# One stage of a fused attention and two-MLP kernel: the attention rounds start their second half one step earlier, and five weight loads move up in a DMA queue

## The chip, the cores and the metric

The kernel runs on one core of one Trainium2 chip. Its time is device microseconds (us) of one execution; the number quoted for a version is the median of its runs. Times "at 158.97" count from the first instruction of the profiled execution.

## What is computed

Three steps follow one another on 4608 tokens of 512 features. `setup_inputs` scales the random inputs; the reference is, cut to what matters:

```python
# attention, separately in every chunk of 64 positions; q, k, v are (8, 8, 576, 64)
scores = matmul(q_c, k_c.T) / sqrt(64)
attn = exp(scores - max(scores)); attn = attn / (sum(attn) + 1e-9)
x = matmul(attn, v_c)                    # -> (4608, 512)
# first MLP, 512 -> 1536 -> 512
x = (sigmoid(x @ w_gate) * (x @ w_val)) @ w_out
# second MLP, 512 -> 2048 -> 512
h = x @ w_in
g = where(h >= 1, h, where(h <= -1, 0, (h + 1) ** 2 / 4))
out = g @ w_out2
```

## The kernel before

All five engines run programs of their own, written out by hand, and meet only at semaphores. Every matmul product is made of three matmuls, since each operand is split into a rounded high part and the low rest.

**First stage** (before 207 us). The first two groups of 384 tokens (t = 0, 1) go through the first MLP with weights that lie in on-chip memory. Per group there are 12 units, and a unit has three **thirds**: a gate product, a val product and an output product, of 12 matmuls each. The steps are numbered `third = (t * C1 + n) * 3 + j`, 0 to 71, and TensorE, ScalarE and VectorE all walk the same numbers. Between the products lie 12 **rounds** of attention (rounds 4 to 15), one for every five thirds. For a round, TensorE makes the scores (`scores`, L649) at the head of a third with `third % 5 == 4`; VectorE subtracts the maximum in that third (`shift`, L1337 and L1340) and divides by the sum in the next (`normalize`, L1348 to L1354); ScalarE takes the exponential (L967). TensorE transposes the probabilities (`transpose_probs`, L660) at `third % 5 == 2`, ScalarE copies them back (`copy_probs_t`, L977), and TensorE multiplies them by v (`mix`, L682) at `third % 5 == 3`. ScalarE then copies the result (`make_x_hi`, L989, in rounds 4 to 7, `save_x`, L1004, in the others) and triggers the next load of v; for rounds 4 to 7 VectorE makes the low part (`make_x_lo`, L1365). In the third with j == 1 VectorE also makes the gated product of the val product of that third (`gated`, L1380 and L1383); its instructions stand in the order shift, normalize, make_x_lo, gated.

**Passes.** From then on 11 passes (MLP1 = 5 of the first MLP, MLP2 = 6 of the second) work on 768 tokens each, with a scheme that makes one product of 2 by 2 blocks out of seven smaller ones. Its operands are sums and differences of blocks: of x (`x_sum`, then `combo_hi` on ScalarE and `combo_lo` on VectorE, L1055 and L1422) and of the weights. A pass has 12 (later 8) units of seven products and then an output stage of 21 (later 28) split pairs (`split_hi` L1145, `split_lo` L1535, TensorE L828 to L830). Passes 0 to 3 carry eight rounds of attention each for the pass behind them. Before the first product of kind 6 of pass 0, TensorE waits for a copy of ScalarE (`copy_chain`, L1068), which stands behind all seven `combo_hi` of that pass in ScalarE's order, and the last of these needs the fourth `x_sum`.

**Weights of the passes.** GpSimd makes the combined and split weights from raw pieces, piece by piece (`prepare`): four operands per piece for the first 18 pieces, 72 in all, each a subtraction (L598), a rounded copy (L605) and the rest (L607). They go into three buffers in turn (from operand 12 on `prep_early`), and from there to device memory. From device memory they come back by loads into a ring of five slots (`load_ring`, L486); two loads make a unit. Ring slots 0 to 4 lie over weights of the first stage, so load n (n < 5) waits for val product 6 + n of t = 1.

All of this is issued by **one queue, SP**, in one written order. `store_prepared` (L452) waits for GpSimd's operand, stores it, and issues loads of the next raw piece before and after (L437). Whatever stands behind a waiting instruction waits too. In pass 0 one load_ring is followed by two, one or two stores, by turns, until all 72 are out (`many`). Load 24 is the first of the output stage of pass 0. The buffers `prep_early` lie where split pairs 2 and 3 are written, so the third `split_hi` of pass 0 waits until every one of the 72 stores has landed.

Of the kernel before, what the change touches and what calls it, by code (L numbers as in the profile page):

```python
# [21 lines left out]
NR = 4  # L22
# [111 lines left out]
def attention_and_mlps(nc, q_k, v, w_gate, w_val, w_out, pieces, out):  # L134
# [4 lines left out]
    with ExitStack() as ctx:  # L139
# [94 lines left out]
        def bank(b):  # L234
            return banks[:, b, 0:N]
# [191 lines left out]
        def _(sp):  # L427
# [88 lines left out]
            for b in (0, 1, 3, 2):  # L516
                load_raw(0, b)
            prepared = 0
            for upto, n in ((35, 0), (38, 1), (41, 2), (44, 3), (46, 4)):
                while prepared < upto:  # L520
                    if prepared % 4 == 0:
                        for _ in range(2 if prepared < 16 else 1):
                            if stored < PIECES_1:
                                store_kept(stored)
                                stored += 1
                    store_prepared(prepared)
                    prepared += 1
                load_ring(0, n)
# [91 lines left out]
        def _(pe):  # L620
# [32 lines left out]
            def transpose_probs(a):  # L653
                way = FIRST[a] if a < NR else FIRST[-1]
                pe.wait_ge(probs_ready, a + 1)
                if 2 <= a < NR:
                    pe.wait_ge(probs_t_copied, a - 1)
                tr = way.tr if a < NR else bank(0)
                for b in range(GROUP // 2):
                    last = pe.transpose(tr[:, b * P:(b + 1) * P], way.probs[:, b * P:(b + 1) * P], ident[:, :])  # L660
                last.then_inc(probs_t_done, 1)
# [243 lines left out]
            for t in range(TILES):  # L905
                for n in range(C1):
                    for j in range(3):
                        third = (t * C1 + n) * 3 + j
                        if third % 5 == 4 and third // 5 < 12:
                            scores(NR + third // 5)  # L910
                        if third % 5 == 2 and 0 < third // 5 <= 12:
                            transpose_probs(NR + third // 5 - 1)
                        if third % 5 == 3 and 0 < third // 5 <= 12:
                            mix(NR + third // 5 - 1)
                        t_next, n_next = t + (n + 1) // C1, (n + 1) % C1
                        if j == 2:
                            add_out(t, n)
                        elif t_next < TILES:
                            (gate, val)[j](t_next, n_next)
                        else:  # L920
                            unit(0, 0, order(0)[j])
# [25 lines left out]
        def _(act):  # L947
# [27 lines left out]
            def copy_probs_t(a, way=FIRST[-1]):  # L975
                act.wait_ge(probs_t_done, a + 1)
                act.activation(way.probs, way.tr if a < NR else bank(0), ACT.Copy).then_inc(probs_t_copied, 1)  # L977
# [217 lines left out]
            for t in range(TILES):  # L1195
                for n in range(C1):
                    for j in range(3):
                        third = (t * C1 + n) * 3 + j
                        if third % 5 == 4 and third // 5 < 12:
                            exponentiate(NR + third // 5)  # L1200
                        if third % 5 == 2 and 0 < third // 5 <= 12:
                            copy_probs_t(NR + third // 5 - 1)
                        if third % 5 == 3 and 0 < third // 5 <= 12:
                            a = NR + third // 5 - 1
                            if a < 2 * NR:
                                make_x_hi(a)
                            else:
                                save_x(a)
                        m = t * C1 + n + 1
                        if j == 0 and m < TILES * C1:  # L1210
                            make_gate(m)
                        if j == 1 and m < TILES * C1:
                            make_g_hi(m)
                        if j == 1 and t == TILES - 1:
                            if n == 6:
                                combo_part(0, 0)
                            if n == 9:
                                combo_part(0, 1)
                            if n == 10:
                                combo_part(0, 2)  # L1220
                                combo_part(0, 3)
                                combo_part(0, 4)
                            if n == 11:
                                combo_part(0, 5)
                                combo_part(0, 6)
                if t == TILES - 1:
                    copy_chain(0, 0, 1)
                save_x2(t)
                store_x2(t)
# [75 lines left out]
        def _(dve):  # L1305
# [269 lines left out]
            for t in range(TILES):  # L1575
                for n in range(C1):
                    for j in range(3):
                        third = (t * C1 + n) * 3 + j
                        if third % 5 == 4 and third // 5 < 12:
                            shift(NR + third // 5)  # L1580
                        if third % 5 == 0 and 0 < third // 5 <= 12:
                            normalize(NR + third // 5 - 1)
                        if third % 5 == 3 and 0 < third // 5 <= NR:
                            make_x_lo(NR + third // 5 - 1)
                        m = t * C1 + n + 1
                        if j == 1 and m < TILES * C1:
# [180 lines left out]
```

## Time and profile before

| what | value |
|---|---|
| median of 3 runs | 1682.48 us (1680.63 to 1684.82) |
| profiled execution: its own time / its span | 1680.63 us / 1678.8 us |
| TensorE busy | 1630.9 us, 97% |
| VectorE, ScalarE, GpSimd busy | 66%, 48%, 26% |
| granted TensorE clock, mean | 0.997 |
| TensorE idle before ring products (L806), 0 to 460 us, for DMA | 5.3 us in 3 waits |

A row of the trace in order of time gives the start, the duration, the engine, the line and the operation, and in brackets how long the engine was idle before it and what released it. Matmuls overlap: each is 0.33 us long, but they start 0.17 us apart at full clock. GpSimd is called POOL, VectorE DVE, ScalarE ACT, TensorE PE, and SPq is the SP queue.

### The profile page before, as it was taken

How to read it: one execution, taken by the hardware profiler on the slowest of the kernel's cores; microseconds unless marked ns; L12 is line 12 of the kernel's file. 1: busy time of each engine (PE TensorE's matmuls, PEld its weight loads, DVE VectorE, ACT ScalarE, POOL GpSimd, SP SyncE). 2: the span in 40 equal slices, each digit the busy share in tenths (PEclk: the TensorE clock that was granted, in tenths of full speed). 3: DMA queues.
4: the chain of work that ended last, by engine and by line, in shares of the span. 5: the costliest groups of instructions: out<-in, count | busy, mean ns of one | idle time of the engine just before them, and what ended most of it. 6: DMA issues, size and time to landing. Idle time of an engine off the chain costs nothing.

```text
span 1678.8 us, 29062 instructions
## 1 busy us (share of the span) xinstructions
PE 1630.9 (97%) x11028; PEld 1586.9 (95%) x11028; DVE 1105.7 (66%) x1607; ACT 805.1 (48%) x1301; POOL 439.3 (26%) x582
## 2 busy tenths in 40 slices
PE   6999999999999999999999999999999999999999
PEld 6999988999989999999999999999999999999999
DVE  5444556576586659456744858669579578688585
ACT  2222333354444445344433556466475475575563
POOL 7877766203460454145134000000000000000000
PEclk9999999999999999999999999999999999999999
DMA  7799899889998998998899887787777787778675
GB/s 193 243 297 322 265 331 337 286 291 326 340 325 298 330 344 309 318 322 320 293 350 330 294 302 286 243 303 284 249 300 278 238 311 267 266 300 277 236 290 171
DMA packets 153386, 489.50 MB, mean 292 GB/s; under 512 B 18080, under 2 KB 68768, under 8 KB 124192
## 3 DMA queue, kind: packets, MB, share of 16 engines
q1 hardware_dynamic: 134368, 457.76, 78.3%
q10 hardware_dynamic: 18880, 29.89, 5.7%
q8 instruction: 88, 1.44, 0.3%
q14 instruction: 50, 0.41, 0.1%
HBM read 406.32 MB, written 81.26 MB: 290 GB/s over the span
## 4 chain that ended last, share of the span: by engine, by line
PE 66%; DMA 11%; POOL 8%; issue 5%; DVE 3%; SPq 1%; ACT 1%; POOLq 0%; DVEq 0%; ACTq 0%
PE banks L806 12%; PE banks L808 11%; PE banks L807 11%; PE banks L828 10%; PE banks L830 10%; PE banks L829 10%; POOL raw L598 3%; POOL prep_early L607 2%; DMA ring<-w_in_split 2%; DMA out_dram<-y 2%; DMA w_in_split<-prep_b 2%; DMA w_in_split<-prep_a 2%; POOL prep_early L605 2%; DMA raw<-pieces_dram 1%; DVE split_lo L1535 1%
## 5 line engine op out<-in xcount | busy, mean ns | idle before, releaser
L806 PE MATMUL banks<-combo_hi,ring 128*128 128x384 f32 x1512 | 519.1, 343 | 18.0 <-DMA ring<-w_in_split 8.6
L808 PE MATMUL banks<-combo_hi,ring 128*128 128x384 f32 x1512 | 507.8, 336 | 0.0
L807 PE MATMUL banks<-combo_lo,ring 128*128 128x384 f32 x1512 | 507.3, 336 | 0.0
L828 PE MATMUL banks<-split_hi,ring 128*128 128x384 f32 x1092 | 366.2, 335 | 6.8 <-DVE split_lo L1535 4.9
L830 PE MATMUL banks<-split_hi,ring 128*128 128x384 f32 x1092 | 364.9, 334 | 0.0
L829 PE MATMUL banks<-split_lo,ring 128*128 128x384 f32 x1092 | 364.9, 334 | 0.0
L806 PEld LDWEIGHTS banks<-combo_hi,ring 128*128 128x128 f32 x1512 | 285.2, 189 | 28.0 <-DMA ring<-w_in_split 11.9
L807 PEld LDWEIGHTS banks<-combo_lo,ring 128*128 128x128 f32 x1512 | 285.4, 189 | 0.0
L808 PEld LDWEIGHTS banks<-combo_hi,ring 128*128 128x128 f32 x1512 | 285.2, 189 | 0.0
L1068 ACT ACTIVATE chain<-banks 128x384 f32<-128x384 f32 x324 | 156.6, 488 | 226.9 <-PE banks L808 221.5
L1535 DVE TENSOR_TENSOR split_lo<-g,split_hi 128x768 fp32r<-128x768 f32 x234 | 231.4, 993 | 35.7 <-ACT split_hi L1145 33.9
L1145 ACT ACTIVATE split_hi<-g 128x768 fp32r<-128x768 f32 x234 | 193.2, 842 | 128.6 <-PE banks L830 69.8
L828 PEld LDWEIGHTS banks<-split_hi,ring 128*128 128x128 f32 x1092 | 205.0, 188 | 10.9 <-issue 9.6
L829 PEld LDWEIGHTS banks<-split_lo,ring 128*128 128x128 f32 x1092 | 205.0, 188 | 0.0
L830 PEld LDWEIGHTS banks<-split_hi,ring 128*128 128x128 f32 x1092 | 205.0, 188 | 0.0
L598 POOL TENSOR_TENSOR raw<-raw 128x256 f32<-128x256 f32 x136 | 116.6, 857 | 54.9 <-DMA raw<-pieces_dram 41.7
L605 POOL CAST prep_a<-raw 128x256 fp32r<-128x256 f32 x56 | 30.9, 552 | 295.0 <-DMA w_in_split<-prep_a 159.4
L1422 DVE TENSOR_TENSOR combo_lo<-x_raw,combo_hi 128x768 fp32r<-128x768 f32 x77 | 78.3, 1019 | 17.0 <-ACT combo_hi L1055 17.0
L1118 ACT ACTIVATE r<-h,half 128x384 f32<-128x384 f32 x48 | 29.6, 617 | 86.6 <-DVE h L1457 86.6
L690 PE MATMUL banks<-x_tile,weights 128*128 128x384 f32 x192 | 67.5, 352 | 0.3 <-DVE x_tile L1359 0.2
L1055 ACT ACTIVATE combo_hi<-x_raw 128x768 fp32r<-128x768 f32 x77 | 63.9, 833 | 3.0 <-issue 3.0
L967 ACT ACTIVATE probs<-probs 128x384 f32<-128x384 f32 x45 | 23.6, 525 | 86.8 <-DVE probs L1340 86.8
(121 smaller groups left out, 2110.1 us busy)
## 6 DMA issues: line engine op xcount, KB each, us to landing
ring<-w_out_split SPq DMA_DIRECT2D x119, 1024.0 KB, 6.6
ring<-w_in_split SPq DMA_DIRECT2D x108, 1024.0 KB, 6.8
ring<-w_in_split SPq DMA_DIRECT2D x108, 768.0 KB, 7.1
ring<-w_out_split SPq DMA_DIRECT2D x35, 512.0 KB, 5.6
raw<-pieces_dram SPq DMA_DIRECT2D x136, 128.0 KB, 5.1
tile_in<-q_k_dram ACTq DMA_DIRECT2D x44, 384.0 KB, 6.2
w_in_split<-weights SPq DMA_DIRECT2D x36, 256.0 KB, 3.7
w_in_split<-prep_early SPq DMA_DIRECT2D x36, 256.0 KB, 3.5
```

The lines of the kernel that those rows point to most:

```text
L598: pool.tensor_tensor(into, *less, op=ALU.subtract).then_inc(prep_summed, 1)
L690: pe.matmul(ps, w_lo, x_hi(par, j), start=(j == 0), stop=False)
L806: pe.matmul(ps, w_lo, hi, start=first and k == 0, stop=False, skip_group_check=more)
L807: pe.matmul(ps, w_hi, lo, start=False, stop=False, skip_group_check=more)
L808: last = pe.matmul(ps, w_hi, hi, start=False, stop=k == 1, skip_group_check=more)
L828: pe.matmul(ps[:, j, :], w_lo, hi, start=first and k == 0, stop=False, skip_group_check=more)
L829: pe.matmul(ps[:, j, :], w_hi, lo, start=False, stop=False, skip_group_check=more)
L830: last = pe.matmul(ps[:, j, :], w_hi, hi, start=False, stop=end, skip_group_check=more)
L1068: act.activation(buf[:, u % 2, :], x_bank(p, u), ACT.Copy).then_inc(copied, 1)
L1145: act.activation(split_hi[:, at % 4], g_part(p, i, kp), ACT.Copy).then_inc(split_hi_ready, 1)
L1422: dve.tensor_tensor(combo_lo[:, i - 1], x_part(i), combo_hi[:, i - 1].bitcast(F32), op=ALU.subtract).then_inc(combo_lo_ready, 1)
L1535: dve.tensor_tensor(split_lo[:, b], g_part(p, i, kp), split_hi[:, b].bitcast(F32), op=ALU.subtract)\
```

## The change

Two edits. On the SP queue, the first five ring loads stand behind 28, 31, 34, 36 and 38 stores of prepared operands instead of 35, 38, 41, 44 and 46; the stores that no longer stand ahead of them follow in pass 0 with the same pattern, which then ends at ring load 25 instead of 20. In the first stage, transposes, mix, the copies behind each and `make_x_lo` move one third earlier; scores, shift, exponential and normalize stay.

```diff
--- before.py
+++ after.py
@@ -516,7 +516,7 @@
             for b in (0, 1, 3, 2):
                 load_raw(0, b)
             prepared = 0
-            for upto, n in ((35, 0), (38, 1), (41, 2), (44, 3), (46, 4)):
+            for upto, n in ((28, 0), (31, 1), (34, 2), (36, 3), (38, 4)):
                 while prepared < upto:
                     if prepared % 4 == 0:
                         for _ in range(2 if prepared < 16 else 1):
@@ -908,9 +908,9 @@
                         third = (t * C1 + n) * 3 + j
                         if third % 5 == 4 and third // 5 < 12:
                             scores(NR + third // 5)
+                        if third % 5 == 1 and 0 < third // 5 <= 12:
+                            transpose_probs(NR + third // 5 - 1)
                         if third % 5 == 2 and 0 < third // 5 <= 12:
-                            transpose_probs(NR + third // 5 - 1)
-                        if third % 5 == 3 and 0 < third // 5 <= 12:
                             mix(NR + third // 5 - 1)
                         t_next, n_next = t + (n + 1) // C1, (n + 1) % C1
                         if j == 2:
@@ -1198,9 +1198,9 @@
                         third = (t * C1 + n) * 3 + j
                         if third % 5 == 4 and third // 5 < 12:
                             exponentiate(NR + third // 5)
+                        if third % 5 == 1 and 0 < third // 5 <= 12:
+                            copy_probs_t(NR + third // 5 - 1)
                         if third % 5 == 2 and 0 < third // 5 <= 12:
-                            copy_probs_t(NR + third // 5 - 1)
-                        if third % 5 == 3 and 0 < third // 5 <= 12:
                             a = NR + third // 5 - 1
                             if a < 2 * NR:
                                 make_x_hi(a)
@@ -1580,7 +1580,7 @@
                             shift(NR + third // 5)
                         if third % 5 == 0 and 0 < third // 5 <= 12:
                             normalize(NR + third // 5 - 1)
-                        if third % 5 == 3 and 0 < third // 5 <= NR:
+                        if third % 5 == 2 and 0 < third // 5 <= NR:
                             make_x_lo(NR + third // 5 - 1)
                         m = t * C1 + n + 1
                         if j == 1 and m < TILES * C1:
```

## Rows read from the trace of the kernel before

**Rows 1.** The page: busy time of each engine, share of the span, instructions.

```profile
PE 1630.9 (97%) x11028; PEld 1586.9 (95%) x11028; DVE 1105.7 (66%) x1607; ACT 805.1 (48%) x1301; POOL 439.3 (26%) x582
```

**Rows 2.** TensorE in time order: start us, us, engine, line, operation.

```profile
39.62 0.33 PE L729 MATMUL banks<-g_hi,weights 128*128 128x384 f32 x1
...
41.70 0.33 PE L690 MATMUL banks<-x_tile,weights 128*128 128x384 f32 x1
```

**Rows 3.** TensorE in time order, at the end of the first stage.

```profile
213.81 0.66 PE L806 MATMUL banks<-combo_hi,ring 128*128 128x384 f32 x1 [2.66 <-DVE combo_lo L1422]
...
220.22 0.40 PE L806 MATMUL banks<-combo_hi,ring 128*128 128x384 f32 x1
```

**Rows 4.** Waits of TensorE, 280 to 320 us: us in total, times, longest.

```profile
PE banks L806 <- DMA ring<-w_in_split: 5.3, 3, 2.0
```

**Rows 5.** TensorE in time order, late in pass 0.

```profile
289.65 0.45 PE L806 MATMUL banks<-combo_hi,ring 128*128 128x384 f32 x1 [1.96 <-DMA ring<-w_in_split]
...
302.55 0.52 PE L808 MATMUL banks<-combo_hi,ring 128*128 128x384 f32 x1
```

**Rows 6.** The SP queue in time order: a store and ring loads.

```profile
163.23 0.33 SPq L452 DMA_DIRECT2D w_in_split<-prep_early  x1
...
181.65 0.33 SPq L486 DMA_DIRECT2D ring<-w_in_split  x1
...
217.21 1.79 SPq L486 DMA_DIRECT2D ring<-w_in_split  x2
```

**Rows 7.** TensorE in time order: scores and transposes of the rounds, waits in brackets.

```profile
43.87 0.58 PE L649 MATMUL banks<-tile_in 64*64 64x64 f32 x24
...
51.57 0.55 PE L660 MATMUL banks<-ident,probs 128*128 128x128 f32 x3 [0.67 <-DVE probs L1354]
...
96.05 0.58 PE L649 MATMUL banks<-tile_in 64*64 64x64 f32 x24 [0.49 <-DVE x_tile L1365]
...
146.44 0.58 PE L649 MATMUL banks<-tile_in 64*64 64x64 f32 x24
...
158.97 0.58 PE L649 MATMUL banks<-tile_in 64*64 64x64 f32 x24
...
165.83 0.49 PE L660 MATMUL banks<-ident,probs 128*128 128x128 f32 x3
```

**Rows 8.** VectorE in time order: probabilities ready, and two gated products.

```profile
99.44 0.75 DVE L1354 TENSOR_TENSOR probs<-probs,row_sum 128x384 f32<-128x384 f32 x1
...
151.36 1.00 DVE L1354 TENSOR_TENSOR probs<-probs,row_sum 128x384 f32<-128x384 f32 x1
...
164.62 0.56 DVE L1354 TENSOR_TENSOR probs<-probs,row_sum 128x384 f32<-128x384 f32 x1
168.52 0.56 DVE L1380 SCALAR_TENSOR_TENSOR g_full<-act_buf,banks 128x384 f32<-128x384 f32 x1 [3.33 <-PE banks L692]
...
198.76 0.55 DVE L1380 SCALAR_TENSOR_TENSOR g_full<-act_buf,banks 128x384 f32<-128x384 f32 x1 [5.83 <-PE banks L692]
```

**Rows 9.** VectorE in time order: the same operation in two stretches.

```profile
207.32 3.98 DVE L1422 TENSOR_TENSOR combo_lo<-x_raw,combo_hi 128x768 fp32r<-128x768 f32 x3
...
339.73 0.95 DVE L1422 TENSOR_TENSOR combo_lo<-x_raw,combo_hi 128x768 fp32r<-128x768 f32 x1
```

**Rows 10.** ScalarE in time order, before TensorE goes on.

```profile
213.20 0.47 ACT L1068 ACTIVATE chain<-banks 128x384 f32<-128x384 f32 x1
```

**Rows 11.** GpSimd in time order: first and last of 24 finished operands.

```profile
229.06 0.73 POOL L607 TENSOR_TENSOR prep_early<-raw,prep_early 128x256 fp32r<-128x256 f32 x1
...
304.32 0.73 POOL L607 TENSOR_TENSOR prep_early<-raw,prep_early 128x256 fp32r<-128x256 f32 x1
```

**Rows 12.** One tile (raw), its DMAs from 220 to 310 us.

```profile
DMA to landing us min/median/max: 3.3/6.3/8.8
```

**Rows 13.** ScalarE in time order, start of the output stage of pass 0.

```profile
330.25 2.32 ACT L1145 ACTIVATE split_hi<-g 128x768 fp32r<-128x768 f32 x3 [2.57 <-DVE g L1469]
```

**Rows 14.** DMA issues, 220 to 310 us: size of one, median us to landing.

```profile
w_out_split<-prep_early SPq DMA_DIRECT2D x24, 256.0 KB, 5.0
```

## Prediction

> **What bounds the kernel now.** I read the page first. TensorE is busy for 97% of the span [rows 1], so only a stop of TensorE, or a spell of its lower clock, can be won or lost. The stages (forty-slice table, windows) put nearly all of its idle time that this change can touch before 330 us. There I read TensorE in order of time, with the idle time ahead of each instruction, and beside it the queues that feed it. Four facts matter.
>
> First, in the first stage TensorE runs without a gap from third to third; a third is twelve matmuls, 41.70 - 39.62 = 2.08 us [rows 2]. Second, where pass 0 begins it stops for 2.66 us and then runs at half rate until 220.22 [rows 3]. Third, late in pass 0 it waits three times for ring loads, 5.3 us in all [rows 4], the first at unit 8 [rows 5]. These loads are late because the SP queue issues them behind stores of prepared operands, and those wait for GpSimd. Fourth, the first ring load goes out at 181.65 [rows 6] although its data is wanted only when pass 0 begins, so loading it earlier is worth nothing by itself. What the edit of the queue really does is change how many stores stand ahead of each later load.
>
> The profiled execution took 1680.63 us (span 1678.8 and 1.8 around it), the lowest of the three; the median is 1682.48. I make the sum against the profiled execution and add it to the median. Differences under 0.3%, some 5 us, are about what a measurement of this kernel cannot tell from none.
>
> **Part 1: transposes, mix and their copies one third earlier.** Per round these are three transposes and 24 small matmuls on TensorE, one copy of the transposed probabilities, two copies of the mix and the trigger of the next v load on ScalarE, and for four rounds two subtractions on VectorE. Nothing is added or removed, so the only price is waiting. The transposes need the probabilities, and VectorE's place for making them does not move.
>
> Today the transposes start 165.83 - 158.97 = 6.86 us after the scores start [rows 7]; one third less leaves 4.78 us. The twelve rounds fall into three kinds, by the place of the scores in the unit of three thirds.
> - Scores ahead of a val product (rounds 4, 7, 10 and 13). VectorE must do the gated product of that val before it normalizes. Probabilities are ready at 164.62 + 0.56 = 165.18, the transposes would be wanted at 158.97 + 4.78 = 163.75: a stop of 1.4 [rows 7, 8]. Three rounds are like this (my readings of the others: 1.4 and 1.5), 4.3 in all. Round 4 is worse: wanted at 43.87 + 4.78 = 48.65, and its transposes start at 51.57, as soon as the probabilities are there [rows 7], so 2.9 instead of the 0.67 paid today, 2.2 more.
> - Scores ahead of the output product (four rounds): wanted at 146.44 + 4.78 = 151.22, ready at 152.36, 1.1 us; the four give 1.1, 1.0, 1.1 and 0.6, so 3.7 in all.
> - Scores ahead of a gate (four rounds): wanted at 96.05 + 4.78 = 100.83, ready at 100.19 [rows 7, 8]. Free, with 0.6 to spare.
>
> TensorE's queue is served in order, so behind the waiting transposes stand the gate, val and output products, and they all move. The mix still comes a third after the transposes, so the 0.5 us copy between them stays hidden: free. If that cover went, each round would pay up to the copy. The earlier mix removes two waits of the scores for x (0.49 of them in [rows 7]) and a small one, 1.0 together. Part 1: +2.2 + 4.3 + 3.7 - 1.0 = **+9.2 us**.
>
> A stop may also cost clock. After the 2.66 stop TensorE ran 18 matmuls in 220.22 - 213.81 = 6.4 us, half of its rate, where 3.1 is the price at the upper level (2.4 GHz): about 3 lost [rows 2, 3]. Round 4's stop would be 2.9 long. But stops of 1.96 and less did not all do this: after 289.65 the rate stayed, and only near 302.55 are there starts 0.32 us apart, about ten of them, 1.5 lost [rows 5]. Bounds for round 4 are 0 and 3; I take **+1.5**, since the nearest row dropped but in a stretch with another wait right behind it. For the 1.0 to 1.5 us stops I take nothing.
>
> **Part 2: the start of pass 0.** After the change SP has issued 28 stores at 163.23 [rows 6] and then waits, in ring load 0, for a val product that ends at about 168.5 [rows 8], now some 8.7 later, at 177. Behind that wait stand the stores, the loads of raw pieces and the kept operands; GpSimd waits for stores (three buffers) and for raw pieces. From there to ring load 4 SP may issue only ten more stores, three per unit. By then (the fifth such val product is over by 198.7 today [rows 8]; plus 9.2 makes 208) 38 are out, and ring load 5 waits for a product of pass 0. So GpSimd should be silent from about 208 to 223.
>
> In that stretch VectorE makes the combinations on which TensorE's 2.66 stop hangs. Three combo_lo took 3.98, 1.33 each, while GpSimd worked; alone one takes 0.95 [rows 9]. ScalarE's chain copy ends at 213.67 [rows 10], behind the last of these sums. Saved with a silent GpSimd: 3 x 0.38 = 1.1, and by the same ratio about 0.8 on the four sums and the product around them. The stop falls to about 0.8, and a stop of 0.8 left the clock alone elsewhere (0.67 in [rows 7]), which gives back the 3. Part 2: **-4.8 us**, between 0 (GpSimd still at work) and -5.7.
> The Trainium skill (SBUF — State Buffer, the part on what actually causes contention) says that VectorE with two SBUF inputs and GpSimd share a port pair as an exclusive lock; the 1.33 against 0.95 here agrees, and by the rule the whole excess would go, as I took it.
>
> **Part 3: ring loads and the end of pass 0.** The three late waits, 5.3, and the 1.5 of clock are gone if loads 16, 18 and 20 come in time: **-6.8 us**. Before load 16 there are now 56 stores instead of 64, and TensorE wants it some 4 us later than today; even at today's pace this works.
>
> But GpSimd has been held back by the same eight stores. Today 24 operands finish between 229.06 and 304.32: 23 steps of 3.27 [rows 11]. After the change SP reaches store 38 at about 224; the next raw piece lands 6.3 later (median, [rows 12]) and operand 40 (counted from 0) is done at about 232.5. Two things then need the last operands. Load 24, the first of the output stage, stands behind store 69. The third split pair writes where the staging buffers lie, so ScalarE waits there until all 72 operands have landed; today it starts at 330.25 [rows 13], after this change it would want to at about 330.25 + 4.4 - 6.8 = 328 (4.4 is 9.2 - 4.8, the shift by then; a fall of the clock in round 4 would move both sides of this comparison).
> - At 3.27 per operand, operand 69 is done at 327.3, its load lands near 333 and was wanted at 324: 9 late, and the last store adds about 1: +10.
> - At 2.91, the pace at which TensorE frees slots (two loads to a unit of some 9.7 us, of which 42 matmuls at 2.08 / 12 are 7.3 and the rest is a round of attention; five stores go to three loads), operand 69 is done at 317 and 71 at 323, landed (5.0, [rows 14]) by 328: nothing is late.
> I take 3.1, nearer to the row: 69 at 322.4, landed 328.5, 4.5 late, and 1 more for the split. **+5.5 us**, between 0 and +10. So the stall goes from unit 8 to the start of the output stage. Passes 1 to 10 are untouched.
>
> **Sum.** 9.2 + 1.5 - 4.8 - 6.8 + 5.5 = **+4.6 us**: the profiled time becomes about 1685, the median 1682.5 + 4.6 = 1687.1.
>
> **Rivals.**
> A. GpSimd keeps pace with the slots, so nothing is late at the end of pass 0: +4.6 - 5.5 = -0.9, 1681.6. For it: GpSimd's own work is only some 2 us per operand. Against: 6.3 for a raw piece in every group of four.
> B. Faster: the silence of GpSimd lasts through more of the first stage, since SP is held from 163 on. VectorE then normalizes sooner: its last operation takes 1.00 in one round and 0.56 in another [rows 8]. If the stops of part 1 fell from 9.2 to 5 and nothing was late at the end, the sum is -0.9 - 4.2 - 1.5 = -6.6, 1676. It decides once part 1 costs under 5. Against it: the stops before 163 us, seven or eight of twelve, lie ahead of that silence, and 1.4 was read with the 0.56.
> C. The clock falls again and again: stops of 1.4 followed by small matmuls bring the lower level in two or three rounds (1.5 to 3 each), and the end of pass 0 is 10 late: 4.6 + 6 + 4.5 = +15, 1697.
> The Trainium skill (TensorE: Matmul & The Clock Gate, the section on oscillation in real kernels) warns that a wait ahead of every tile can leave the clock throttled each time; here the row at 213.81 agrees and the one at 289.65 does not.
> D. The edit of the queue does nothing, because load 0 was never late: then parts 2 and 3 vanish, +9.2 + 1.5 = 10.7, 1693. Against it: the wait in load 0 surely reorders the stores.
>
> **Chances.** My sum 0.48; A 0.20; B 0.10; C 0.12; D 0.10. The sum's own range is 1684 to 1691, of which about half lies over 1687.5. Faster by over 0.3% (under 1677.4) comes from B alone: 0.10. Within 0.3%: A and 0.22 of the sum, 0.42. Slower: the rest of the sum, C and D, 0.48. For 8 in 10 the range reaches from the edge of B to beyond C: 1677.5 to 1698.
>
> **What would show it.** TensorE's transposes wait for VectorE's probabilities in eight of twelve rounds, 1 to 1.5 us each and near 3 in the first; the granted clock dips there or not. GpSimd is idle for some 15 us before pass 0, combo_lo takes 0.95 there, and the 2.66 stop shrinks. The ring waits at units 8 to 10 are gone, and there is a wait for a ring load or a split pair where the output stage of pass 0 starts. I am wrong if the probabilities come sooner than read, if GpSimd is not silent, or if the output stage starts without a wait.

## The result, and the profile after

| version | median, us | runs |
|---|---|---|
| before | 1683.65 | 4 (1680.63 to 1691.88) |
| after | 1709.07 | 4 (1704.60 to 1709.46) |

The ratio (of the means) is 1.0137, with a 95% interval of 1.0097 to 1.0177: the change makes the kernel some 23 us slower. That is the side I held likeliest, but five times the size that I worked out, and outside my range. The profiled execution of after took 1708.61 us. Two later executions, one of e4 (4088.33 us) and one of e5 (3438.33 us), took more than twice as long as the others and count in no median below. The top of its page (engine, busy us, share of the span, instructions) stands against [rows 1]:

```profile
span 1706.8 us, 29062 instructions
PE 1641.1 (96%) x11028; PEld 1594.0 (93%) x11028; DVE 1103.7 (65%) x1607; ACT 805.6 (47%) x1301; POOL 437.6 (26%) x582
```

TensorE's busy time grew by 1641.1 - 1630.9 = 10.2 us with the same 11028 matmuls. No work was added, so these are matmuls that ran longer, at the lower clock above all: behind 40 us the granted clock stood at half for 23.9 us in all, before for 10.2. The rest of the 28 us between the two spans is idle time.

**Where it comes from.** I marked the start of the same steps in both traces; the difference of the starts is the shift.

| step | before | after | shift | second trace of after |
|---|---|---|---|---|
| first ring product of pass 0 | 206.83 | 222.45 | +15.6 | +12.9 |
| past the stop at the start of pass 0 | | | +12.4 | +9.4 |
| output stage of pass 0 | 326.2 | 346.3 | +20.1 | +16.6 |
| output stage of pass 1 | 477.2 | 505.9 | +28.7 | +16.2 |
| output stage of pass 3 | 782.6 | 811.8 | +29.2 | +20.9 |
| end | 1678.8 | 1706.8 | +28.0 | +22.1 |

The second trace is of a later execution, e9 below. Of the +15.6, 2.1 was there before the first moved instruction (TensorE's lower clock at the very start lasted until 34.1 us instead of 29.2), so it is no part of the change. And the profiled execution of before is one of its fastest: of 72 timed beside the experiments two took less than its 1680.63, and their medians are 1685.75 to 1687.71. So some 5 of the 28 us are not the change's either.

**First stage.** The view of lines, all of it before 222 us, groups TensorE's transposes (busy us, mean ns of one, idle us before them and what ended it):

```profile
L660 PE MATMUL banks<-ident,probs 128*128 128x128 f32 x39 | 7.2, 296 | 12.4 <-DVE probs L1354 12.4
```

In before the same wait was 0.67 in round 4 [rows 7] and nothing in the other rounds. The waits are eight, and three of them, with the lower clock behind the first, look like this in TensorE's order of time:

```profile
53.36 0.55 PE L660 MATMUL banks<-ident,probs 128*128 128x128 f32 x3 [2.46 <-DVE probs L1354]
...
54.64 0.52 PE L692 MATMUL banks<-x_tile,weights 128*128 128x384 f32 x1
54.96 0.52 PE L690 MATMUL banks<-x_tile,weights 128*128 128x384 f32 x1
...
137.22 0.55 PE L660 MATMUL banks<-ident,probs 128*128 128x128 f32 x3 [2.51 <-DVE probs L1354]
...
177.99 0.55 PE L660 MATMUL banks<-ident,probs 128*128 128x128 f32 x3 [1.33 <-DVE probs L1354]
```

Starts 0.32 us apart instead of the 0.17 of [rows 2] are the lower level of the clock. It lasted for 7 matmuls there, and did not come behind the equally long stop at 137.22. What VectorE did ahead of the transposes at 81.66 (round 6) and 137.22, in its order of time, against [rows 8]:

```profile
80.13 1.47 DVE L1354 TENSOR_TENSOR probs<-probs,row_sum 128x384 f32<-128x384 f32 x1
...
136.17 0.99 DVE L1354 TENSOR_TENSOR probs<-probs,row_sum 128x384 f32<-128x384 f32 x1
```

The same division takes 0.56 in other rounds. At 136 us GpSimd was running one subtraction and copy after another. Round 13 stops for 1.33 although GpSimd was idle from 169.9 to 195.0 and its division took 0.56: that stop is the place of the normalize alone, as predicted.

**Start of pass 0.** TensorE in order of time, against [rows 3]:

```profile
228.48 0.41 PE L806 MATMUL banks<-combo_hi,ring 128*128 128x384 f32 x1 [1.70 <-ACT chain L1068]
...
230.02 0.41 PE L806 MATMUL banks<-combo_hi,ring 128*128 128x384 f32 x1 [0.26 <-DVE x_tile L1392]
...
231.59 0.41 PE L806 MATMUL banks<-combo_hi,ring 128*128 128x384 f32 x1 [0.28 <-ACT chain L1068]
```

The 2.66 stop became 1.70 and two short ones, and the clock stayed up. VectorE's three combinations, against [rows 9], took 0.90 each:

```profile
223.46 2.69 DVE L1422 TENSOR_TENSOR combo_lo<-x_raw,combo_hi 128x768 fp32r<-128x768 f32 x3
```

This is because GpSimd is silent just then. Its operand 39, its next start and operand 40, in its own order of time:

```profile
222.01 0.74 POOL L607 TENSOR_TENSOR prep_early<-raw,prep_early 128x256 fp32r<-128x256 f32 x1
...
238.16 0.74 POOL L598 TENSOR_TENSOR raw<-raw 128x256 f32<-128x256 f32 x1 [15.41 <-DMA raw<-pieces_dram]
...
239.65 0.73 POOL L607 TENSOR_TENSOR prep_early<-raw,prep_early 128x256 fp32r<-128x256 f32 x1
```

**End of pass 0.** TensorE's ring products and the first product of the output stage, against [rows 4, 5]:

```profile
312.60 0.44 PE L806 MATMUL banks<-combo_hi,ring 128*128 128x384 f32 x1 [3.31 <-DMA ring<-w_in_split]
...
323.80 0.44 PE L806 MATMUL banks<-combo_hi,ring 128*128 128x384 f32 x1 [2.08 <-DMA ring<-w_in_split]
...
334.08 0.44 PE L806 MATMUL banks<-combo_hi,ring 128*128 128x384 f32 x1 [1.17 <-DMA ring<-w_in_split]
...
346.31 0.66 PE L828 MATMUL banks<-split_hi,ring 128*128 128x384 f32 x1 [4.67 <-issue]
346.77 0.52 PE L829 MATMUL banks<-split_lo,ring 128*128 128x384 f32 x1
347.09 0.52 PE L830 MATMUL banks<-split_hi,ring 128*128 128x384 f32 x1
```

Three ring waits remain, 6.6 us, and a stop of 4.67 stands where the output stage begins, with half rate until 351.6. "issue" says only that no releaser was found. It was the first load of that stage: it went out here (SP's queue) and landed 5.4 us later, at 346.2, just before TensorE went on:

```profile
340.78 0.38 SPq L486 DMA_DIRECT2D ring<-w_out_split  x1
```

The last of the 72 operands and the third `split_hi` (GpSimd's and ScalarE's rows, against [rows 11, 13]):

```profile
344.66 0.72 POOL L607 TENSOR_TENSOR prep_early<-raw,prep_early 128x256 fp32r<-128x256 f32 x1
```

```profile
349.88 0.84 ACT L1145 ACTIVATE split_hi<-g 128x768 fp32r<-128x768 f32 x1 [6.98 <-DMA w_out_split<-prep_early]
```

The last operand comes 40.3 us later than before. In pass 1, further waits follow, the largest of them this one, with half the clock until 501.7 us:

```profile
495.81 0.69 PE L806 MATMUL banks<-combo_hi,ring 128*128 128x384 f32 x1 [2.92 <-DMA ring<-w_in_split]
```

The load that ended it went out at 486.8, again behind a slow producer. The queue stood from 475.6 to 480.3 for an operand of GpSimd, and GpSimd for the landing of an earlier store (in its own order of time):

```profile
478.09 0.74 POOL L605 CAST prep_a<-raw 128x256 fp32r<-128x256 f32 x1 [6.30 <-DMA w_in_split<-prep_a]
```

### The profile page after: what moved, and what is told of

It reads as the page before. It is cut to its first block, busy times and chain, and to the rows that moved or that the text cites. A ratio compares the mean times of both kernels' runs of the same rounds, so it can differ in the third digit from the quotient of the medians.

```text
span 1706.8 us, 29062 instructions
## 1 busy us (share of the span) xinstructions
PE 1641.1 (96%) x11028; PEld 1594.0 (93%) x11028; DVE 1103.7 (65%) x1607; ACT 805.6 (47%) x1301; POOL 437.6 (26%) x582
## 4 chain that ended last, share of the span: by engine, by line
PE 70%; DMA 13%; POOL 5%; issue 5%; DVE 4%; ACT 1%; ACTq 1%; SPq 1%; POOLq 0%; DVEq 0%
PE banks L806 10%; PE banks L828 10%; PE banks L830 10%; PE banks L829 10%; PE banks L807 10%; PE banks L808 10%; DMA w_in_split<-prep_a 2%; DMA out_dram<-y 2%; DMA ring<-w_in_split 2%; DMA w_out_split<-prep_b 2%; DMA w_out_split<-prep_a 2%; PE banks L690 2%; POOL raw L598 2%; POOL prep_early L607 1%; PE banks L692 1%
## 5 line engine op out<-in xcount | busy, mean ns | idle before, releaser
L1535 DVE TENSOR_TENSOR split_lo<-g,split_hi 128x768 fp32r<-128x768 f32 x234 | 232.4, 997 | 40.3 <-ACT split_hi L1145 38.7
L690 PE MATMUL banks<-x_tile,weights 128*128 128x384 f32 x192 | 68.3, 356 | 0.3 <-DVE x_tile L1359 0.2
L692 PE MATMUL banks<-x_tile,weights 128*128 128x384 f32 x192 | 65.7, 342 | 0.0
L691 PE MATMUL banks<-x_tile,weights 128*128 128x384 f32 x192 | 65.4, 341 | 0.0
```

The lines of the kernel that those rows point to most:

```text
L690: pe.matmul(ps, w_lo, x_hi(par, j), start=(j == 0), stop=False)
L692: return pe.matmul(ps, w_hi, x_hi(par, j), start=False, stop=(j == KT - 1))
L1535: dve.tensor_tensor(split_lo[:, b], g_part(p, i, kp), split_hi[:, b].bitcast(F32), op=ALU.subtract)\
```

## The experiments

Theory F (the prediction's mechanisms with larger sizes): the move costs stops of TensorE in the first stage, and the queue edit gives GpSimd a silence that it pays back at the end of pass 0. Its rivals: the queue edit is harmless and everything is the move (R1), or most of the loss arises only when both edits are together (R2). Medians are over 9 to 11 runs (5 for e5, 4 for e11), ratios are of means, beside runs of the kernel before on the same chip (medians 1685.75 for e1 to e4, 1687.19 for e5 to e8, 1687.71 for e11 and e12).

| run | median, us | ratio to before, 95% |
|---|---|---|
| e1 queue edit alone | 1689.49 | 1.0020 [0.9991, 1.0048] |
| e2 move alone | 1693.33 | 1.0041 [1.0017, 1.0065] |
| e3 move, normalize earlier | 1688.61 | 1.0021 [0.9999, 1.0043] |
| e4 before, fewer stores in pass 0 | 1681.55 | 0.9976 [0.9953, 0.9999] |
| e5 after again | 1707.17 | 1.0129 [1.0105, 1.0153] |
| e6 the hold alone | 1692.15 | 1.0022 [1.0005, 1.0039] |
| e7 queue edit, eight stores ahead of load 5 | 1689.88 | 1.0008 [0.9988, 1.0028] |
| e8 e4 and an earlier chain copy | 1680.27 | 0.9955 [0.9937, 0.9972] |
| e11 after, eight stores ahead of load 5 | 1705.58 | 1.0097 [1.0059, 1.0134] |
| e12 after, normalize earlier | 1695.74 | 1.0049 [1.0029, 1.0070] |

**e1: the queue edit alone.**

```diff
-            for upto, n in ((35, 0), (38, 1), (41, 2), (44, 3), (46, 4)):
+            for upto, n in ((28, 0), (31, 1), (34, 2), (36, 3), (38, 4)):
```

> Before, with only the edit of the SP queue (28, 31, 34, 36, 38 stores ahead of ring loads 0 to 4). Theory: the ring loads 0 to 4 hold the queue at times set by TensorE, so GpSimd is silent before pass 0 whether or not the attention moves. The stop at the start of pass 0 shrinks from 2.7 to about 1.5 without the lower clock (3 to 5 us won), but operand 71 ends near 325 instead of 305 and the ring loads of units 8 to 11 and of the output stage come late: 6 to 12 us lost. Sum +2 to +8 us, ratio 1.001 to 1.005. Rival, my prediction's part 3: the late loads come in time and only the output stage waits, sum about -5 us, 0.997. Rival, the queue edit alone is nearly the whole loss: +20 us, 1.012.

The output stage of pass 0 starts at 331.87, 5.6 later than before, and the trace ends 8.0 later. From the first ring product (205.75) to the output stage it is 126.1 us, before 119.4, so +6.7. TensorE from 205 to 350 us, by lines, and in order of time:

```profile
L806 PE MATMUL banks<-combo_hi,ring 128*128 128x384 f32 x168 | 61.1, 364 | 9.6 <-DMA ring<-w_in_split 7.9 <-ACT chain L1068 1.4 <-DVE x_tile L1392 0.3
```

```profile
211.47 0.41 PE L806 MATMUL banks<-combo_hi,ring 128*128 128x384 f32 x1 [1.40 <-ACT chain L1068]
...
331.87 0.66 PE L828 MATMUL banks<-split_hi,ring 128*128 128x384 f32 x1 [4.76 <-issue]
```

Both ends of the mechanism are there without the move: the smaller stop at the start of pass 0, the stop at its end. And the ring waits are not fewer but more, 7.9 us in four instead of 5.3 in three. R1 falls by the trace; the timed ratio alone could not tell this edit from none.

**e2: the move alone.**

```diff
-                        if third % 5 == 2 and 0 < third // 5 <= 12:
+                        if third % 5 == 1 and 0 < third // 5 <= 12:
                             transpose_probs(NR + third // 5 - 1)
-                        if third % 5 == 3 and 0 < third // 5 <= 12:
+                        if third % 5 == 2 and 0 < third // 5 <= 12:
                             mix(NR + third // 5 - 1)
```

(and the same for ScalarE's copies and VectorE's `make_x_lo`; the five counts as before).

> Before, with only the attention moves. Theory: the transposes wait for the probabilities in eight rounds, 12 us in all with some clock, so TensorE reaches pass 0 about 13 us later; but GpSimd, which nothing holds, is then 13 us further ahead, and the late ring waits of 5.3 us and their 1.5 of clock go. Sum +5 to +8 us, ratio 1.004. Rival, costs simply add: the moves alone cost about 13 to 15 us over the whole run, 1.008. Rival, the moves are nearly the whole loss: +20 us, 1.012.

Its transposes, by lines, before 222 us:

```profile
L660 PE MATMUL banks<-ident,probs 128*128 128x128 f32 x39 | 7.6, 308 | 13.0 <-DVE probs L1354 12.9
```

Eight waits again, 12.9 us, and half rate behind two of them (from 94.8 and from 136.9). Pass 0 begins at 222.59, +15.8, and its output stage 115.8 us later, 3.6 sooner than before. So the stops are the move's own. The end is +10.5. I had expected the late ring waits to go; they did not (5.6 us in three). What was won, 3.8 us, was won at the start of pass 0, where the stop on the chain copy was only 1.16 with the queue's counts untouched. GpSimd and VectorE there, each in order of time:

```profile
237.92 1.11 POOL L598 TENSOR_TENSOR raw<-raw 128x256 f32<-128x256 f32 x1 [16.05 <-DMA raw<-pieces_dram]
```

```profile
223.06 2.70 DVE L1422 TENSOR_TENSOR combo_lo<-x_raw,combo_hi 128x768 fp32r<-128x768 f32 x3
```

So GpSimd was silent here too: TensorE arrives later, and ring load 5 holds the queue from 215.9 to 231.3 with 46 stores out instead of 38. The last operand still comes at 316.27, and nothing stops at the output stage.

**e3: the move, and VectorE's normalize right behind shift, ahead of the gated product.**

```diff
                             shift(NR + third // 5)
-                        if third % 5 == 0 and 0 < third // 5 <= 12:
-                            normalize(NR + third // 5 - 1)
+                            normalize(NR + third // 5)
```

> The attention moves alone, and VectorE normalizes right behind the shift, ahead of the gated product. Theory: in rounds 4, 7, 10 and 13 the gated product stood between, so their stops (2.5, 1.8, 2.5 and 1.3 in the changed kernel) vanish and only the four stops of rounds 6, 9, 12 and 15 (1.5, 0.5, 1.3, 1.0) stay: waits of the transposes fall from about 12 to 4 us, and the run is 5 to 9 us faster than with the moves alone. Rival, the stops come from slow VectorE operations beside GpSimd: they shrink little, under 3 us in all.

The waits left are four, 4.4 us in all, in the rounds ahead of an output product; this is TensorE in order of time:

```profile
75.30 0.55 PE L660 MATMUL banks<-ident,probs 128*128 128x128 f32 x3 [1.36 <-DVE probs L1354]
...
114.26 0.55 PE L660 MATMUL banks<-ident,probs 128*128 128x128 f32 x3 [1.20 <-DVE probs L1354]
...
154.31 0.55 PE L660 MATMUL banks<-ident,probs 128*128 128x128 f32 x3 [0.74 <-DVE probs L1354]
...
193.24 0.55 PE L660 MATMUL banks<-ident,probs 128*128 128x128 f32 x3 [1.07 <-DVE probs L1354]
```

The long stops of rounds 4, 7, 10 and 13 are gone. It was the gated product standing ahead of normalize that made them, as the prediction said. One wait of the mix for its copy (1.46) is new. Pass 0 starts at 211.32, 4.5 late instead of 15.8. The median is 4.7 us under e2's, a little less than the 5 to 9 expected, and the two intervals overlap.

**e4: the kernel before, with four stores to three ring loads in pass 0 in place of five.**

```diff
-                    many = min(2 if n % 3 else 1, MADE_1 - prepared)
+                    many = min(1 if n % 3 else 2, MADE_1 - prepared)
```

> Before, with four stores to three ring loads in pass 0 instead of five (the 72nd then stands at ring load 24). Theory: ring loads 16, 18 and 20 were late because GpSimd's 3.3 us per operand cannot keep up with five stores per three loads; with four it must deliver one in 3.6 us, so the three waits of 5.3 us and the 1.5 of clock go, and all 72 are out before the third split needs the buffers: -5 to -8 us, ratio 0.996. Rival: the raw pieces, loaded from the same queue, are slowed by as much and the wait moves to the output stage: 0 to +5 us.

In pass 0 two ring waits are left, 0.63 and 2.60, of the three in [rows 4]; the output stage starts 3.7 earlier. Then pass 1 has a ring wait of 3.12, and the trace ends 3.3 later than before's. The timed runs say 4 us faster. So stores ahead of loads are what makes loads late in pass 0, but a good part of what is won there can be lost in the next pass.

**e5: after, run again.**

> The changed kernel unchanged, on the chip of this group of runs. Theory, the costs of the two edits add: queue edit +0.2%, moves +0.4% by their medians, so +0.6%, some 1695 us, and the 1.4% of the first measurement held a disturbance. Rival, the edits make each other worse (held GpSimd, later TensorE, and pass 1 starts with waits of its own): ratio 1.011 to 1.015 again, and the same +6 us between the output stages of passes 0 and 1.

1707.17, and the ratio of 1.0129 is the 1.0137 of the first four runs within the intervals. So the theory, that the two costs add, fails.

**e6: the hold alone.** The loads stay where they were, but the queue waits at store 28, 31, 34, 36 and 38 for the val products for which loads 0 to 4 would have waited there.

```diff
                 while prepared < upto:
+                    held = {28: 7, 31: 8, 34: 9, 36: 10, 38: 11}.get(prepared)
+                    if held:
+                        sp.wait_ge(val_done, C1 + held)
```

> Before, with the ring loads where they were, but the SP queue waits for the five val products at stores 28, 31, 34, 36 and 38. Theory: these five waits are the smaller part of the hold, GpSimd ends its 72 operands near 312 instead of 305 (330 with the queue edit), and TensorE's waits for ring loads grow by 1 to 4 us. Rival, these waits are the hold: the end is near 325 to 330 and the run is as slow as with the queue edit.

The last operand is finished at about 310.6, only 6 later than before's 304.32, and there is no stop at the output stage; ring waits 2.41, 1.24 and 4.68. In time it costs as much as e1 (1.0022 and 1.0020). So e1's late end of the operands comes from load 5 and not from these five waits, but the time does not tell the two edits apart.

**e7: the queue edit, with the eight stores put back ahead of ring load 5** (stores 38 to 45; so load 5's wait for a product of pass 0 no longer stands in front of them).

```diff
                 load_ring(0, n)
+            while prepared < 46:
+                if prepared % 4 == 0 and stored < PIECES_1:
+                    store_kept(stored)
+                    stored += 1
+                store_prepared(prepared)
+                prepared += 1
```

> The queue edit alone, and eight more stores between ring loads 4 and 5, so that 46 stand ahead of load 5 as before. Theory: the hold that matters is load 5, which waits for a product of pass 0 with only 38 stores out (GpSimd silent for 15 us): the 72 operands end near 310, the ring waits and the 4.8 us stop of the output stage fall back to 5 us or less, while the stop at the start of pass 0 is again 2.5 or more, since GpSimd works beside VectorE: between 0 and +3 us against before, 3 to 6 faster than the queue edit alone. Rival, the five early waits hold it: no difference from the queue edit alone.

The last operand and TensorE's two large waits, each in order of time (lines from here on count six more than in before):

```profile
306.26 0.73 POOL L613 TENSOR_TENSOR prep_early<-raw,prep_early 128x256 fp32r<-128x256 f32 x1
```

```profile
213.96 0.66 PE L812 MATMUL banks<-combo_hi,ring 128*128 128x384 f32 x1 [2.97 <-DVE combo_lo L1428]
...
271.74 0.69 PE L812 MATMUL banks<-combo_hi,ring 128*128 128x384 f32 x1 [4.64 <-DMA ring<-w_in_split]
```

This separates the two halves of the queue edit. The last operand is back from 330.12 in e1 to 306.26, and the stop at the output stage is gone. The stop at the start of pass 0 is back as well, 2.97, since GpSimd now works through it. In e1 both the gain and the loss come from load 5 waiting with only 38 stores out; e2 has the gain with 46 out and no such loss, so the silence helps VectorE, and the eight missing operands are what the end of the pass pays for. A stop of 4.64 has appeared elsewhere, at 271.74, since load 5 now stands behind the eight stores, and the time is no better than e1's within the intervals (1.0008 and 1.0020).

**e8: e4, and ScalarE's chain copy and the saving of x ahead of the last two combinations.** TensorE's stop at the start of pass 0 hangs on that copy [rows 10].

```diff
                             if n == 11:
-                                combo_part(0, 5)
-                                combo_part(0, 6)
+                                copy_chain(0, 0, 1)
                 if t == TILES - 1:
-                    copy_chain(0, 0, 1)
+                    combo_part(0, 5)
                 save_x2(t)
+                if t == TILES - 1:
+                    combo_part(0, 6)
```

> Four stores to three ring loads in pass 0, and at the end of the first stage ScalarE copies the first chain, and both engines save the second group's output, ahead of the last two combinations. Theory: the 2.7 to 3.2 us stop at the start of pass 0 hung on these orders; it falls under 1 us and the lower clock behind it (3 us) goes: 4 to 6 us less than with four stores alone, ratio to before 0.993 to 0.995. Rival, the saves only push the combinations back and TensorE stops at product 4 or 3 of unit 0 instead: no gain over 0.9976.

The stop shrinks and no half rate follows it; this is TensorE in order of time, against [rows 3] and the 3.23 that e4 has there:

```profile
213.04 0.41 PE L806 MATMUL banks<-combo_hi,ring 128*128 128x384 f32 x1 [1.82 <-DVE x_tile L1393]
```

I had expected under 1 us for the stop and a ratio of 0.993 to 0.995. At 1680.27 against 1687.19 the two edits together are 0.45% faster than before and 1.7% faster than e5's after. Against e4's 0.9976 the second edit's share is not clear of noise: the intervals overlap.

**e9 and e10: one more profiled execution each of after and before.**

> The changed kernel once more, for a second profile. Theory, its extra loss over the sum of the two edits lies where the first trace has it: stop of 4 to 5 us at the first split of pass 0, and then waits in pass 1 that shift TensorE by another 5 to 8 us between the first two output stages. Rival, the waits of pass 1 come and go from run to run and this trace has them elsewhere or not at all.

> The kernel before once more, for a second profile. Its first profiled execution, 1680.6, is 5 us under the usual 1686. Theory: the 5 us are one or two more late ring loads with a spell of the lower clock behind them, in pass 0 or 1; the first stage is the same within 2 us. Rival: the whole trace is stretched evenly.

1702.75 and 1680.24. The stops are there again in e9 (11.8 us at the transposes; ring waits of 8.9 us, from unit 8 on; 2.01 at the output stage), with other sizes, and behind those of the first stage and of the output stage the clock stayed up. Pass 1 loses nothing there, so the rival of e9 holds. After's two traces differ by up to 12.5 us (the table above). Before's two agree within 2.1 us at every output stage, but both are among its fastest executions, so e10 could not show where the usual 1686 loses its 5 us. The first trace of after, 1708.61, is close to the median, and e9's is below all nine timed runs of after (1704.60 to 1715.14).

**e11: after, with e7's stores ahead of load 5.**

> The changed kernel with eight more stores between ring loads 4 and 5. Theory: the silence of GpSimd at load 5 is what the queue edit costs, also on top of the moves: operands end near 325 instead of 345, the stop at the output stage goes, and the run comes down to the cost of the moves alone plus at most 4 us, ratio 1.004 to 1.006. Rival, the loss over the sum is in pass 1 or later and not from the queue: 1.010 to 1.013.

The last operand is done at 323.49 instead of 344.66 and nothing stops at the output stage, as in e7. But the stop at the start of pass 0 is 2.74 again, four ring waits sum to 10.7, and the median is 1705.58: I had expected 1.004 to 1.006 and got 1.0097. The same us are lost earlier: between 255 and 290 us, behind the eight stores, the shift grows from 12.8 to 21.4, and it is 20.5 at the output stage, where after has 20.1. This half of the queue edit is worth little in time, in after as in e1.

**e12: after, with e3's normalize.**

> The changed kernel with VectorE normalizing ahead of the gated product. Theory, costs of the moves add to those of the queue edit: 5 to 9 us less than the changed kernel, ratio 1.008 to 1.010. Rival, TensorE's earlier arrival at pass 0 only meets the held operands sooner: the same 1.013.

1695.74, 0.49% over before, where I had expected 0.8 to 1.0%. e1 and e3 together would give 0.41%, so with the earlier normalize the two edits add, and 0.8% of after's 1.3% hangs on the order in which VectorE works: the earlier normalize takes 4.7 us from e2 and some 12 from after. The stop at the output stage is there unchanged (337.20, 5.11).

**What the runs leave open.** Up to the output stage of pass 0 the two edits add in the traces: e1's 5.6 and e2's 12.1 are 17.7, and after has 20.1 and 16.6. At the end they do not: 8.0 + 10.5 = 18.5 against 28.0 and 22.1, and by the timed ratios 0.61% against 1.3%. (Each of these shifts is against a fast execution of before, some 5 us under its median, and a sum of two counts that twice; so the traces make the gap look smaller than it is.) What is missing lies in passes 1 and 2 in the traces (waits for v at 438 and 477 us and for a ring load at 496 in the first; in the second pass 1 loses nothing and pass 2 loses 4.6). So R2 holds for a part of the loss, 4 to 10 us by the traces and about 12 by the timed runs, half of the whole. Why the two together cost that was not found, and e12 shows only that it goes when the long stops go.

## Why the prediction was wrong, step by step

**Part 1, +9.2 and +1.5 of clock: right mechanism, too small.** Eight of twelve rounds stop, in the places named, and the four ahead of a gate are free. I had 1.4 or so for rounds 7, 10 and 13 and 2.9 for round 4; measured from scores to transposes they are 1.94, 2.67, 1.49 and 2.62, and rounds 6, 9, 12 and 15 give 1.68, 0.62, 1.49 and 1.16. The probabilities' own operation had been read as 0.56 in a round where VectorE ran alone; beside GpSimd it takes up to 1.47, and others ahead of it likewise. The eight sum to 13.7 instead of the prediction's 11 or so. Less the 0.7 paid before and the 1.0 of removed waits, and with one spell of lower clock (7 matmuls by 0.15, 1.1), that makes 13.1; the trace has 15.6 - 2.1 = 13.5, and I had 10.7.

**Part 2, -4.8: right in the mechanism, its cause half seen.** GpSimd was silent (15.4 us), combo_lo fell to 0.90, the stop to 1.70 (2.24 with its two small successors; I had 0.8) and the clock stayed: 12.4 - 15.6 = -3.2. With GpSimd at work through that stretch e7 has the long stop back, 2.97. The Trainium skill (SBUF — State Buffer, the section on who interferes with whom) has VectorE and GpSimd share a port pair as an exclusive lock; 1.33 against 0.90 agrees. But I gave the queue edit the credit for the silence, and e2 shows that the move brings it as well: GpSimd was silent for 16.05 us with the counts untouched, and the shift fell by 3.8.

**Part 3, -6.8 and +5.5: the step that failed.** "If loads 16, 18 and 20 come in time ... even at today's pace this works" looked only at the wait of unit 8. That wait did go in the first trace (e9 has 1.87 there, and e1 1.57). But the pace that carries the loads is that of the stores between them, and the stores wait for an operand each. All of GpSimd's work starts later: operand 40 came at 239.65, not 232.5, since the shift behind the stop was 12.4 where I had 4.4, and from there to operand 71 it took (344.66 - 239.65) / 31 = 3.39 each, not 3.1. So in units 9 to 11 the ring loads were late again, and with them the output stage. From the end of the first stop to behind the start of the output stage the shift grows by 10.1 (12.4 to 22.55), where I had -1.3: three waits that I had taken away (5.3 before, 6.6 after), two spells of lower clock (about 1.6 each) where before had one, and at the output stage 4.67 and another 2.4 of clock. The term that failed most is thus the -6.8: it measured +2.9, while the end of the pass cost 7.1 instead of 5.5. I had treated the release of unit 8 and the delay of the end as two effects that add. They are one queue with one slow producer: giving a load precedence over eight stores puts the delay of those stores on every load behind them. What this is worth in time is less sure than where it shows: by the timed runs the queue edit alone (e1) costs 0.2%, no clear difference, and e7 and e11, which take the stop at the output stage away, gain little.

**"Passes 1 to 10 are untouched": wrong.** By the output stage of pass 2 or 3 another 4 to 6 us are lost in both traces (22.55 to 28 in the first, 16.6 to 20.9 in the second). From pass 3 to the end it changes by -1.2 and +1.3. At least the load that was late in pass 1 of the first trace stood in the same queue behind the same producer.

**The rivals.** C (the clock falls again and again, and the end of pass 0 is 10 late; 1697) comes nearest: the clock fell behind the stop of round 4, twice in the ring, at the output stage and in pass 1. The Trainium skill (TensorE: Matmul & The Clock Gate, the section on oscillation in real kernels) warns of this pattern; only one of the eight stops of the first stage brought it here. D (the edit of the queue does nothing; 10.7 for the move alone) is refuted by the traces of e1 and e7, though not by their times, A (GpSimd keeps pace) by the last operand at 344.66, B (a faster first stage) by the 12.4 us of waits at the transposes. The range was too narrow because even C, its dearest case, had the three ring waits gone and nothing lost behind pass 0.

## What to carry to other kernels

When loads move up in a queue served in order, list what now stands behind each of their waits, and follow the slowest producer among it to its last deadline: here eight postponed stores moved the last operand back by 26 us (e1) and, by the traces, cost some 10 us at 310 to 350 us; put back right ahead of load 5 (e11) they cost about as much at 255 to 290. Before a consumer moves a step earlier, compare, round by round, when its input is ready with when it would be wanted, take the durations from rounds where the shared engines are both busy, and move the producer with it: e3's earlier normalize took the price of this move from 15.8 to 4.5 us at the start of pass 0.

## What the runs showed of the hardware

- A stop of TensorE brought the lower clock in some places and not in others: 2.46 (round 4) was followed by 7 matmuls at half rate and 3.31 by about ten, 4.67 by fifteen, but 2.51 (round 10) and 1.70 by none. In e2 round 10's stop did bring it, in e9 it did not. In the thirteen traces used here, behind the first 36 us, the granted clock was halved during or within 3 us of all 27 stops from 2.6 to 5.1 us, but only at 18 of the 55 stops from 1.7 to 2.5. So for such a stop one trace does not tell what it costs.
- The same VectorE instruction (128x384, two inputs in on-chip memory) took 0.56 us in all 35 cases where no GpSimd instruction overlapped it, and 0.56 to 1.50 in the 121 where one did: 1.47 at 80.13 us of after, but 0.56 at 126.83 of before.
- One kernel's executions differ in where they lose: two of after are up to 12.5 us apart in pass 1. The two traces of before agree within 2.1 us at the output stages, but its 31 timed runs beside e1 to e4 spread over 16.5 us (1678.79 to 1695.30), so two traces do not show a kernel's spread.
